# Fused channel attention and two MLPs on one core: squares by the tile in six PSUM banks with two running sums, four chunks split by GpSimd alone and used out of order, warm-up on a constant, both single tiles first

## The reference

```
qn = q / (norm(q, axis=tokens) + 1e-6)          # q, k: [6016, 256]
kn = k / (norm(k, axis=tokens) + 1e-6)
s  = kn.T @ qn / tau                            # 256 x 256, over channels
a  = exp(s - max) ; a /= a.sum(-1) + 1e-9
x  = v @ a                                      # [6016, 256]
x  = relu(x @ w_in) ** 2 @ w_out                # first MLP
y  = leaky_relu(x @ w_in2, 0.01) @ w_out2       # second MLP
```

## Time and profile before

| what | value |
|---|---|
| median of 3 runs | 1029.77 us (1029.61 to 1029.98) |
| time of the profiled execution | 1031.27 us |
| its span | 1029.5 us, 13098 instructions |
| TensorE (PE) busy | 1023.3 us, 99% |
| VectorE (DVE) busy | 723.6 us, 70% |
| ScalarE (ACT) busy | 669.7 us, 65% |
| GpSimd (POOL) busy | 18.1 us, 2% |

### The profile page before, as it was taken

How to read it: one execution, slowest core, us unless ns; L and a number is a source line. 1 busy time by engine, 2 the same in 40 slices (tenths; PEclk the granted TensorE clock), 3 DMA queues, 4 the chain that set the end, 5 groups by cost and what they waited for, 6 DMA issues and landing times.

```text
span 1029.5 us, 13098 instructions
## 1 busy us (share of the span) xinstructions
PE 1023.3 (99%) x4606; PEld 861.3 (84%) x4606; DVE 723.6 (70%) x1184; ACT 669.7 (65%) x1155; POOL 18.1 (2%) x25
## 2 busy tenths in 40 slices
PE   9999999999999999999999999999999999999998
PEld 8887888888888888888888888888888888888887
DVE  5898867667667667666556767777777777867665
ACT  6788877777767767777766555555556556565554
POOL 1500000000000000000000000000000000000000
PEclk9999999999999999999999999999999999999999
DMA  9711020140132131123443002002002002000001
GB/s 365 262 56 31 22 90 32 67 136 31 67 96 71 59 106 65 52 98 132 169 153 118 1 1 81 1 1 80 1 1 80 1 1 81 1 1 24 17 0 42
DMA packets 33731, 69.26 MB, mean 67 GB/s; under 512 B 2690, under 2 KB 18562, under 8 KB 33666
## 3 DMA queue, kind: packets, MB, share of 16 engines
q1 hardware_dynamic: 33090, 67.25, 18.9%
q10 hardware_dynamic: 576, 1.18, 0.3%
HBM read 44.56 MB, written 23.86 MB: 66 GB/s over the span
## 4 chain that ended last, share of the span: by engine, by line
PE 95%; DMA 1%; DVE 1%; ACT 1%; issue 0%; ACTq 0%; SPq 0%; DVEq 0%
PE psum L510 31%; PE psum L512 31%; PE psum L511 31%; PE psum L517 2%; DMA qk<-in_k 1%; DVE xop_lo L1046 0%; DVE g_lo L1150 0%; ACT g_hi L850 0%; DVE sq_sum L1004 0%; ACT psum L731 0%; DVE sq_sum L1019 0%; ACT folded L837 0%; ACT win_hi L784 0%; DVE wout_lo L1127 0%; DVE g L1157 0%
## 5 line engine op out<-in xcount | busy, mean ns | idle before, releaser
L850 ACT ACTIVATE g_hi<-g 128x496 fp32r<-128x496 f32 (+1 forms) x384 | 237.2, 618 | 204.1 <-DVE g L1160 76.6
L1150 DVE TENSOR_TENSOR g_lo<-g,g_hi 128x496 fp32r<-128x496 f32 (+1 forms) x384 | 259.9, 677 | 132.0 <-ACT g_hi L850 129.5
L510 PE MATMUL psum<-g_hi,wout_hi 128*128 128x496 f32 (+1 forms) x768 | 296.1, 386 | 0.0
L512 PE MATMUL psum<-g_hi,wout_lo 128*128 128x496 f32 (+1 forms) x768 | 296.1, 386 | 0.0
L511 PE MATMUL psum<-g_lo,wout_hi 128*128 128x496 f32 (+1 forms) x768 | 296.0, 385 | 0.0
L510 PE MATMUL psum<-xop_hi,win_hi 128*128 128x496 f32 (+1 forms) x672 | 259.4, 386 | 0.7 <-ACT psum L928 0.7
L511 PE MATMUL psum<-xop_lo,win_hi 128*128 128x496 f32 (+1 forms) x672 | 259.1, 386 | 0.0
L512 PE MATMUL psum<-xop_hi,win_lo 128*128 128x496 f32 (+1 forms) x672 | 259.1, 386 | 0.0
L510 PEld LDWEIGHTS psum<-g_hi,wout_hi 128*128 128x128 f32 x768 | 144.2, 188 | 27.4 <-issue 0.3
L512 PEld LDWEIGHTS psum<-g_hi,wout_lo 128*128 128x128 f32 x768 | 144.2, 188 | 27.3
L511 PEld LDWEIGHTS psum<-g_lo,wout_hi 128*128 128x128 f32 x768 | 144.2, 188 | 27.1
(11 more groups left out here) (104 smaller groups left out, 674.4 us busy)
## 6 DMA issues: line engine op xcount, KB each, us to landing
up_parts<-park_up SPq DMA_DIRECT2D x8, 896.0 KB, 4.3
qk<-in_q SPq DMA_DIRECT2D x15, 384.0 KB, 9.7
qk<-in_k SPq DMA_DIRECT2D x13, 384.0 KB, 11.5
stage_o<-in_w_out SPq DMA_DIRECT2D x16, 256.0 KB, 3.3
down_parts<-park_down SPq DMA_DIRECT2D x8, 512.0 KB, 2.9
raw<-in_vT SPq DMA_DIRECT2D x8, 496.0 KB, 4.8
x_tiles<-out_buf SPq DMA_DIRECT2D x8, 496.0 KB, 2.8
raw<-x_tiles SPq DMA_DIRECT2D x8, 496.0 KB, 4.3
```

The lines of the kernel that those rows point to most:

```text
L510: pe.matmul(out, a_hi, b_hi, start=start and i == 0, stop=False, **more)
L512: last = pe.matmul(out, a_lo, b_hi, start=False, stop=stop and i == len(operands) - 1, **more)
L850: act.activation(g_hi[:, tile, 0:W], g[:, tile, 0:W], ACT.Copy).then_inc(g_hi_made[tile], 1)
L1150: dve.tensor_tensor(g_lo[:, tile, 0:W], g[:, tile, 0:W], g_hi[:, tile, 0:W].bitcast(F32), ALU.subtract).then_inc(g_split[tile], 1)
```

## The change

Five things change, all but the last in the first stage.

1. **Squares.** ScalarE squares one tile at a time into one of six banks; VectorE adds each tile to one of two running sums in turn (45 adds of 512 columns where there were 28 of 768 and 2 of 512), and ends with one add of the two sums (two before).
2. **Splits.** Four chunks are split (5, 8, 10, 12) where there were three (7, 10, 13). GpSimd makes copy and subtraction of all of them (ScalarE made the first copy before), each chunk in a place of its own. TensorE takes the chunks in the order 0, 1, 2, 3, 4, 6, 7, 5, 9, 11, 8, 10 and then 13, 14, 12 as the tail.
3. **Edges.** Both single tiles are loaded first and multiplied first; before, the second was loaded behind chunk 2 and multiplied last in either half. Their squares start the running sums.
4. **Warm-up.** Six matmuls on a constant of the program's start, where there were seven on `ones` that GpSimd writes.
5. **Window 2.** ScalarE's `x_high(1, 1)` stands in window 2 ahead of `keep_u2`, where it stood near the end of window 1 (window 0 is the first).

```diff
-SPLIT_CHUNKS = (7, 10, 13)
-SPLIT_SLOTS = 2
-SQ_SLOTS = 2
-TAIL_CHUNKS = 3
+MAIN_CHUNKS = (0, 1, 2, 3, 4, 6, 7, 5, 9, 11, 8, 10)
+TAIL_CHUNKS = (13, 14, 12)
+SPLIT_CHUNKS = (5, 8, 10, 12)
 EARLY_CHUNKS = 2
-WARM_UP = 7
+SQ_BANKS = 6
+WARM_UP = 6
 CHUNK = 1024
...
-        sq_sum = at("sq_sum", [P, 2, QK_TILES, C], F32, o_xh0 + 49152)
-        edge = at("edge", [P, 2, EDGES, C], F32, o_xh0 + 55296)
-        qk_hi = at("qk_hi", [P, SPLIT_SLOTS, 2, QK_TILES, C], F32R, o_wout_hi)
-        qk_lo = at("qk_lo", [P, SPLIT_SLOTS, 2, QK_TILES, C], F32R, o_wout_hi + SPLIT_SLOTS * 6144)
+        sq_sum = at("sq_sum", [P, 2, 2, C], F32, o_xh0 + 49152)
+        edge = at("edge", [P, EDGES, 2, C], F32, o_xh0 + 55296)
+        split_places = (o_win_hi + 7168, o_win_lo + 7168, o_wout_hi, o_wout_hi + 12288)
+        qk_hi = [at(f"qk_hi{n}", [P, 2, QK_TILES, C], F32R, o) for n, o in enumerate(split_places)]
+        qk_lo = [at(f"qk_lo{n}", [P, 2, QK_TILES, C], F32R, o + 6144) for n, o in enumerate(split_places)]
...
-        sq = [psum[:, 3 * i:3 * i + 3, :].rearrange("p a x -> p (a x)").rearrange(
-            "p (i t c) -> p i t c", i=2, c=C) for i in range(SQ_SLOTS)]
+        sq = [banks[i].rearrange("p (i c) -> p i c", i=2) for i in range(SQ_BANKS)]
...
+        USED_ORDER = MAIN_CHUNKS + TAIL_CHUNKS
+        assert sorted(USED_ORDER) == list(range(QK_CHUNKS)) and TAIL_CHUNKS[-1] in SPLIT_CHUNKS
+        def wait_used(engine, c):
+            if c != USED_ORDER[-1]:
+                engine.wait_ge(chunk_used, USED_ORDER.index(c) + 1)
+            else:
+                engine.wait_ge(gram_ready, CB)
+        def wait_taken(engine, c):
+            if c in SPLIT_CHUNKS:
+                engine.wait_ge(chunk_split, QK_TILES * (SPLIT_CHUNKS.index(c) + 1))
+            else:
+                wait_used(engine, c)
...
                 if c >= QK_SLOTS:
-                    sp.wait_ge(chunk_used, c - QK_SLOTS + 1)
-                    sp.wait_ge(squared, squares_at(c - QK_SLOTS) + 1)
+                    wait_taken(sp, c - QK_SLOTS)
+                    sp.wait_ge(squared, squares_of(c - QK_SLOTS))
                 for i, src in enumerate((q_t, k_t)):
...
-            sp.dma_start(edge[:, 0, 0, :], q_t[:, 0, :]).then_inc(edge_loaded[0], 16)
+            for t in range(EDGES):
+                sp.dma_start(edge[:, t, 0, :], q_t[:, t, :]).then_inc(edge_loaded[t], 16)
             for c in range(EARLY_CHUNKS):
                 sp.dma_start(qk[:, c, 0, :, :], q_t[:, chunk_tokens(c), :]).then_inc(qk_loaded[c], 16)
             for c in range(EARLY_CHUNKS, QK_CHUNKS):
-                if c == EDGES_AFTER:
-                    load_edge(1)
                 load_chunk(c)
                 if c == QK_SLOTS - 1:
...
-                    if n == 0:
-                        pool.wait_ge(chunk_hi, 1)
-                    else:
-                        pool.wait_ge(tile_hi, QK_TILES * (n - 1) + t + 1)
-                    pool.tensor_tensor(qk_lo[:, place, :, t, :], qk[:, slot, :, t, :], qk_hi[:, place, :, t, :].bitcast(F32),
+                    pool.wait_ge(tile_hi, QK_TILES * n + t + 1)
+                    pool.tensor_tensor(qk_lo[n][:, :, t, :], qk[:, slot, :, t, :], qk_hi[n][:, :, t, :].bitcast(F32),
                                        ALU.subtract).then_inc(chunk_split, 1)
-                if n > 0:
-                    pool.wait_ge(qk_loaded[slot], 32 * (c // QK_SLOTS + 1))
-                if n >= SPLIT_SLOTS:
-                    pool.wait_ge(chunk_used, SPLIT_CHUNKS[n - SPLIT_SLOTS] + 1)
+                pool.wait_ge(qk_loaded[slot], 32 * (c // QK_SLOTS + 1))
                 for t in range(QK_TILES):
-                    if n > 0:
-                        pool.tensor_copy(qk_hi[:, place, :, t, :], qk[:, slot, :, t, :]).then_inc(tile_hi, 1)
+                    pool.tensor_copy(qk_hi[n][:, :, t, :], qk[:, slot, :, t, :]).then_inc(tile_hi, 1)
                     if t > 0:
                         low(t - 1)
                 low(QK_TILES - 1)
...
-            pe.wait_ge(constants, 1)
+            fill = nc.const_aps.tensor(1.0, [P, P], F32)
             for i in range(WARM_UP):
-                pe.matmul(gram[0][:, 0:P], ones[:, :], ones[:, :], start=True, stop=True)
-            pe.wait_ge(edge_loaded[0], 32)
-            for b in range(CB):
-                gram_half(b, edge[:, 0, 0, :], edge[:, 1, 0, :], True, False)
-            for c in range(QK_CHUNKS - TAIL_CHUNKS):
+                pe.matmul(gram[0][:, 0:P], fill, fill, start=True, stop=True)
+            for t in range(EDGES):
+                pe.wait_ge(edge_loaded[t], 32)
+                for b in range(CB):
+                    gram_half(b, edge[:, t, 0, :], edge[:, t, 1, :], t == 0, False)
+            for c in MAIN_CHUNKS:
...
-            for c in range(QK_CHUNKS - TAIL_CHUNKS, QK_CHUNKS):
+            for c in TAIL_CHUNKS:
                 wait_chunk(c)
-                if c == QK_CHUNKS - 1:
-                    pe.wait_ge(chunk_added, 2 * (QK_CHUNKS - 1))
+                if c == TAIL_CHUNKS[-1]:
+                    pe.wait_ge(constants, 1)
                     pe.wait_ge(tau_loaded, 16)
+                    pe.wait_ge(chunk_added, TILES + 1)
                     pe.matmul(tau_bc, ones[:, :], tau_in[:, :], start=True, stop=True).then_inc(tau_ready, 1)
-                    pe.wait_ge(chunk_added, 2 * QK_CHUNKS + QK_TILES - 1)
                     for i in range(2):
                         for b in range(CB):
-                            total = pe.matmul(sums[:, i, b, :], sq_sum[:, i, 0, b * P:(b + 1) * P], ones[:, 0:2],
+                            total = pe.matmul(sums[:, i, b, :], sq_sum[:, 0, i, b * P:(b + 1) * P], ones[:, 0:2],
                                               start=True, stop=True)
                     total.then_inc(sums_ready, 1)
                 for t in range(QK_TILES):
-                    gram_chunk(0, c, t)
-            pe.wait_ge(edge_loaded[1], 32)
-            gram_half(0, edge[:, 0, 1, :], edge[:, 1, 1, :], False, True).then_inc(gram_ready, 1)
+                    last = gram_chunk(0, c, t)
+            last.then_inc(gram_ready, 1)
             for b in range(CB):
                 pe.wait_ge(diag_ready, b + 1)
...
-            for c in range(QK_CHUNKS - TAIL_CHUNKS, QK_CHUNKS):
-                if c == QK_CHUNKS - 1:
+            for c in TAIL_CHUNKS:
+                if c == TAIL_CHUNKS[-1]:
                     transposes(0)
                 for t in range(QK_TILES):
                     last = gram_chunk(1, c, t)
-                last.then_inc(chunk_used, 1)
-            gram_half(1, edge[:, 0, 1, :], edge[:, 1, 1, :], False, True).then_inc(gram_ready, 1)
+                last.then_inc(gram_ready if c == TAIL_CHUNKS[-1] else chunk_used, 1)
...
-            act.dma_start(edge[:, 1, 0, :], k_t[:, 0, :]).then_inc(edge_loaded[0], 16)
+            for t in range(EDGES):
+                act.dma_start(edge[:, t, 1, :], k_t[:, t, :]).then_inc(edge_loaded[t], 16)
...
-            def squares(j, held, tiles):
-                if j > SQ_SLOTS:
-                    act.wait_ge(chunk_added, 2 * (j - SQ_SLOTS))
-                place = sq_sum if j == 0 else sq[(j - 1) % SQ_SLOTS]
-                act.activation(place[:, :, 0:tiles, :], held, ACT.Square).then_inc(squared, 1)
+            for t in range(EDGES):
+                act.wait_ge(edge_loaded[t], 32)
+            act.activation(sq_sum[:, :, :, :], edge[:, :, :, :], ACT.Square).then_inc(squared, 1)
             for c in range(QK_CHUNKS):
-                if c == EDGES_AFTER:
-                    for t in range(EDGES):
-                        act.wait_ge(edge_loaded[t], 32)
-                    squares(EDGES_AFTER, edge[:, :, :, :], EDGES)
                 slot = c % QK_SLOTS
                 act.wait_ge(qk_loaded[slot], 32 * (c // QK_SLOTS + 1))
-                if c == SPLIT_CHUNKS[0]:
-                    act.activation(qk_hi[:, 0, :, :, :], qk[:, slot, :, :, :], ACT.Copy).then_inc(chunk_hi, 1)
-                squares(squares_at(c), qk[:, slot, :, :, :], QK_TILES)
+                for t in range(QK_TILES):
+                    m = c * QK_TILES + t
+                    if m >= SQ_BANKS:
+                        act.wait_ge(chunk_added, m - SQ_BANKS + 1)
+                    act.activation(sq[m % SQ_BANKS], qk[:, slot, :, t, :], ACT.Square).then_inc(squared, 1)
             def weights_hi(n):
                 held, hi, _ = wi1_chunk(n)
...
+                if Q == 2:
+                    x_high(1, 1)
+                    keep_u2(Q)
                 if G == 0 and quad < QUADS - 1:
                     up_sums_high(quad + 1)
-                if Q > 1:
+                if Q > 2:
                     keep_u2(Q)
...
-                if Q == 1:
-                    x_high(1, 1)
                 g_high(Q, C21)
...
-            def add_squares(j, tiles):
-                dve.wait_ge(squared, j + 1)
-                for i in range(2):
-                    if j > 1:
```

(25 more changed lines are left out.)

34 lines of the change are left out of this document (18 added, 16 removed).

## The result

The changed kernel takes 1031.21 us (median of 22 runs, 1028.71 to 1032.66), the kernel before 1029.36 in the same comparison (22 runs, 1028.60 to 1030.05): ratio 1.0015, 95% interval 1.0008 to 1.0021. The forecast was 1026.3 with a range up to 1028.2. The change was to win 3.5 us and loses 1.9: the interval leaves out 1, so it is slower, by 0.15%.

What follows compares the result with a forecast made beforehand. TensorE was taken as the bound, busy 1023.3 of 1029.5 us, with gains in the first 50 us. Tail -2.8 and window 2 -0.85 sum to -3.65, taken as -3.5: 1029.77 - 3.5 = 1026.3 us, range 1025.4 to 1028.2.

Steps and rivals of the forecast that it cites:

- Start: Ahead of chunk 0: 256 KB more to load cost 0.65 us, so chunk 0 starts at about 6.35 instead of 5.71.
- That delay is no loss in itself: Chunk 0's later start, at about 6.35, costs nothing, since the next gate is later.
- just in time: Up to chunk 11: TensorE gets there at about 29.5, as it lands at 29.49, so start shifts of tenths change little.
- Tail: After chunk 11: sums start at 39.0 without waiting, half 0's transposes at 44.65 instead of 47.42, -2.8 us.
- Behind the transposes: End of half 1: TensorE's extra 0.7 us is not kept, since the fold waits for VectorE; 2.8 counted, 3.5 possible.
- Window 2: TensorE's wait for the seed goes once x_high(1, 1) stands behind it: -0.85 us, bounds 0 and 0.85.
- Fourth split: In the tail's -2.8: 0.5 us for the fourth split chunk, less the clock's share in the rest.
- the two positions: Start of half 0's transposes, 44.65 forecast against 47.42 before; said to hold all of the -2.8 us.
- Costed at nothing: Counted at no cost: ScalarE's 30 more squares, `down_high(0)` waiting for half 1, weights' high parts, load order but for the edge.
- A row and a rule: Final add of the two sums beside GpSimd's chunk 12: by the row no wait, by the rule one subtraction's wait.
- The rival's mechanism: GpSimd holds up the final add by up to 1.25 us; about 0.9 lost, -2.6, 1027.2; chance 0.15.
- The rival on the other side: Start: a 0.35 us gap behind the shorter warm-up keeps TensorE at 1.2 GHz, 0.5 lost per us; chance 0.05.

Runs made afterwards that it cites:

- experiment 2: The kernel before, with both halves of the second single tile loaded right behind the first's on both queues and nothing else: 1033.20 us against 1029.29.
- experiment 4: The changed kernel, with eight constant matmuls more between the single tiles and chunk 0: 1030.77 us, ratio 1.0015 to the kernel before.
- experiment 7: The kernel before, with only the q half of the second tile moved first, on SyncE's queue: 1031.76 us against 1029.48.
- experiment 6: The changed kernel, with both single tiles in one transfer per tensor, rows of 2 KB: 1029.59 us, ratio 0.9994 to the kernel before.
- experiment 11: experiment 1 with the second tile's loads behind chunk 0 instead of chunk 2, each half in the changed kernel's queue: 1027.48 us, ratio 0.9974.
- experiment 1: The changed kernel, with the second tile's loads and products moved back behind chunk 2: 1027.46 us, ratio 0.9979 to the kernel before.
- experiment 3: The kernel before, with only x_high(1, 1) moved into window 2: 1028.70 us against 1029.29, ratio 0.9998.
- experiment 12: experiment 1 without the move in window 2, x_high(1, 1) back in window 1: 1028.23 us against 1029.49 for the kernel before.
- experiment 8: experiment 1 with the old warm-up, seven matmuls on ones behind GpSimd's constants: 1027.44 us, ratio 0.9979 to the kernel before.
- experiment 10: experiment 6 with nine warm-up matmuls instead of six: 1027.71 us, ratio 0.9980 to the kernel before.
- experiment 9: experiment 1 with chunk 12 not split, so three split chunks: 1027.04 us, ratio 0.9975 to the kernel before.
- experiment 5: The changed kernel, with the k half of the second tile on SyncE's queue instead of ScalarE's: 1030.60 us against 1029.48 for the kernel before.

## Why the prediction was wrong, step by step

- **Start: the step that failed.** The forecast took chunk 0's delay from bytes, 256 KB at the steady rate, 0.65 us, and put it at 6.35; it came at 9.40, 3.05 later. With a second 1 KB-row transfer directly behind the first in both queues, the loads run at 270 to 310 GB/s from 3 to 7 us instead of 380 to 420 (the changed kernel, experiment 2, experiment 4), and with the pair in one queue (7), in one transfer (6) or apart (11) they don't. TensorE runs dry for 2.37 us, and then works at 1.2 GHz until about 13.3, for 1.67 us more over the 84 records. The transposes are late by about the sum of the two, 3.05 + 1.67 = 4.7: 49.06 - 44.65 = 4.4. Experiments 1 and 2 price the order at 3.75 and 3.9. Of the 4.9 us between forecast and measurement (1031.21 - 1026.3) this step is 3.75; the other 1.16 (1027.46 - 1026.3) stand under the tail. Why the large rows are slow behind two small transfers in each queue (the number of transfers, their 1 KB rows, the addresses in DRAM) no run tells: experiment 6 changed number and rows together. It stays open.
- **"That delay is no loss in itself"** was a part of the same step. In the old order it holds in the one profile there is: experiment 7's execution starts 1.0 us late and has its transposes no later (what its median loses is another matter, not shown). In the new order nothing is left that TensorE waits for: in the changed kernel it works without a wait from chunk 0 to the end, so idle time at the start goes on to the end. The change had taken away the slack that the sentence counted on. Meeting chunk 11 "just in time" was true only for the start that the forecast had assumed.
- **Tail: the order of events right, its worth too high.** With the second tile late the sums start at 39.05 (39.0) and the transposes at 44.57 (44.65). But the -2.8 counted 1.65 for the clock of the earlier trace rows, read from an execution that took 1031.27 where the median of 22 is 1029.36 and the highest 1030.05. Such executions exist, but they are few: of the 97 of the kernel before that ran beside the experiments, 14 have a mean granted clock of 0.998 (1030.37 to 1031.82 us). Experiment 3 shows before's order without that fall, transposes at 45.60. From there the tail wins 1.0, and the fold starts at 45.93 in experiment 1, at 47.42 in experiment 3, 1.5 us; the times give 1.26 (experiment 12). I had corrected the level of the forecast for that execution's 1.5 us and still left its clock term in the gain: the same 1.5 us counted twice. Corrected, the forecast would have been 1026.3 + 1.65 = 1027.95, and experiment 1 measured 1027.46.
- **Behind the transposes:** taken as not kept. The fold's gain of 1.5 lies between the 1.0 of the transposes and what TensorE's own 0.7 more would give, so some of it was kept.
- **Window 2: right.** -0.85 in the sum, 0.77 measured (0.6 in experiment 3), and the wait is gone.
- **Fourth split: wrong.** It stood for some 0.5 in the tail. By the prediction's own terms only half 0 of chunk 12 stands ahead of the transposes, 1.05 us for 1.31, so 0.26 was the most it could give there; kernels with and without it take 1027.46 and 1027.04. The parts named for the -2.8 (1.65, 0.9, 0.5, and 0.88 less 0.65 for the start) add up to 3.3, ahead of a share that it left without a number; the forecast followed the two positions.
- **Costed at nothing:** the warm-up on a constant (experiment 8), squares by the tile, and the two running sums gave no loss that shows. Warm-up products being fewer was harmless only with data at 3.6: in experiment 6, where the first product on data starts at 4.46, three more are worth 1.4 to 1.9 us (experiment 10).
- **A row and a rule: I chose the wrong one.** The Trainium skill (SBUF — State Buffer, "Who interferes with whom") lets a two-input SBUF add of VectorE and a GpSimd instruction that reads SBUF exclude each other. The final add takes 0.69 us with GpSimd idle (experiment 9), 1.06 in experiment 1 and 1.77 in the changed kernel, and it ends 0.55 us behind GpSimd's last subtraction wherever that is: 41.46 and 40.91 in the changed kernel, 38.78 and 38.24 in experiment 1. Here too the trace agrees with the rule, but for a part: behind a full wait the add would end 0.69 behind the subtraction, and it ends 0.55 behind. The row that spoke against it had an overlap of 0.13 us only, and its add ended 0.56 behind the subtraction, as the long overlaps do. The exclusion cost no time in any of the three, since TensorE came to the sums later, and 0.2 us in experiment 12, where TensorE did wait for the add. The rival's mechanism was right, its price not.
- **The rival on the other side** was a slow start. Its sign and its clock were right, its cause was not: not the shorter warm-up, but the loads. It had 0.05. Two of the signs of being wrong that the prediction named came: the edges' eight records take 3.38 us, until 7.03, and the final add ends at 41.46. Of the signs of being right, the sums waited for nothing and the clock was 1.00 from 40 to 50; the tail did what it was to do, 4.4 us late.

The lowest median is that of experiment 9, the whole change but for the second tile's place and the fourth split: 1027.04 us, 2.5 under the kernel before. The intervals of the ratios don't part it from experiments 1, 8 and 11.

## What to carry to other kernels

The first transfers of a kernel aren't priced by their bytes: look at when each lands, and before small transfers are put ahead of the large ones, ask whether the engine that runs dry has any wait left further on that makes the delay good. Where it has none, as here, the idle time and the lower clock behind it go on to the end. Before a fall of the clock is put into a sum, see whether the profiled execution stands above the median by just that much; an event of one execution in seven isn't in the median. In the same way a profile that stands a microsecond or two below its kernel's median (experiments 4, 5, 6 and 7) doesn't show what the typical execution loses. Here small blocks of one tensor did better in one transfer, and a warm-up that reached to the first data did better than one that ended 0.8 us ahead of them.

## What the runs showed of the hardware

- Two 128 x 1 KB transfers in a row on both queues, ahead of 3 KB-row ones: 303 and 272 GB/s (3 to 5 and 5 to 7 us) at a DMA share of 0.91 and 0.90, against 386 and 418 at 0.98 and 1.04 with one. The engines are busy nearly all the same, so the share doesn't tell a slow transfer from a fast one; the GB/s column does. In 5 to 7 us it is the large rows that are slow, 0.16 us a packet against 0.12, when the small ones are past.
- Equal starts come up to speed at different times. The four records of the first tile start at 4.14 behind the same warm-up in the kernel before and in experiment 7, and take 1.15 and 1.91 us; the eight of both tiles take 3.38 us in the changed kernel and 2.18 in experiment 4, whose program is the same up to there. In the first microseconds the granted clock is shown as 1.00 while the warm-up's records take 0.24 us each (2.90 / 12), against 0.12 for the same products in experiment 4's filler (1.95 / 16); the duration of a record is the better witness there.
- Not every idle stretch of TensorE near the start is followed by the 1.2 GHz level: it was behind 2.37 us (changed kernel), 3.31 (experiment 2) and 1.94 (5), and not behind 0.69 (7), 0.97 (11) and 1.43 (4), one execution each.
- An add of VectorE with both inputs in SBUF that overlaps GpSimd's subtraction ends 0.55 to 0.56 us behind it in the kernel before, the changed kernel and every experiment but the ninth, where nothing overlaps (39.26 behind 38.71 in experiment 10, 39.15 behind 38.60 in experiment 11, 39.44 behind 38.87 in the kernel before). Alone it takes 0.69.
